# TensorE's job loop entered once with its body skipped, and sixteen turns of the identity at layer 2's begin

## The chip, the cores and the metric

The kernel runs on one core of a Trainium2 chip, as one launch. The metric is the device time of that core in microseconds (us). TensorE, VectorE (DVE), ScalarE (ACT), GpSimd (POOL) and SyncE (SP) each run their own list of instructions and meet at semaphores; TensorE's rows come as PE (matmuls), PEld (weight loads) and a sequencer (rows with q) that waits, branches and loads registers.

## The reference

Three stages, each feeding the next:

```
attention:  q, k of 4 x 12 heads, 448 tokens, 64 wide, RMS-normed; softmax(q k^T / 8) v
            -> x, 1792 tokens x 768
experts:    logits = cos(x, expert_emb) / tau; expert = argmax of 8; gate = its softmax share
            out[mask_e] = gate * (relu(x[mask_e] @ w1[e]) @ w2[e])      # 768 -> 1024 -> 768
layer 2:    (sigmoid(x @ w_gate) * (x @ w_val)) @ w_out                 # 768 -> 1536 -> 768
```

How many tokens an expert gets is known only when attention and routing have run. All is in float32; the kernel makes each product from three products of a high and a low part.

## The kernel before

Each stage is a block: every engine has its own code in it, and all five meet at a barrier between blocks. `attention` (lines 183 to 1040) works through 24 pairs of heads. GpSimd makes its constants (`constants`, line 150) inside this block, one after the other with a wait on each; TensorE there opens with 52 turns of the identity (line 874).

`experts` (line 1198) begins with VectorE's `job_table`, some twenty small instructions that turn the counts per expert into a list of jobs. A job is up to 294 tokens (T) of one expert; there are between 8 and 14 of them, so the loops over jobs have a length that is loaded from the table. Each engine's `jobs` waits for `table_ready` and loads that number. VectorE then clears six PSUM banks (`banks_set`) and waits for `tokens_turned`; TensorE turns the list of tokens (line 1571), VectorE copies it out (line 1476), which releases `tokens_out`, and then scales the gathered rows of the first job (line 1497). TensorE turns these rows into the first job's x (line 1578), ScalarE and VectorE split it into XH and XL, and the first product of line 1539 can start.

TensorE's loop (line 1582) holds the job's code twice: once with 256 columns (TS) for a short job, once with 294 (T) for a long one, 306 matmuls each, one behind the other in its code. `long_job` loads a flag from the table; two branches choose. Behind a short job, the branch of line 1586 skips the whole long body to reach the loop's end.

`layer2` (line 1591) computes gate and value by seven products of half-blocks (Strassen-like), with TensorE's `product` (three products of line 1984 to 1986 for each of three blocks). Its first products wait for BH and BL, the split tokens, that ScalarE and VectorE make block by block; VectorE's adds of line 1793 (`common` and the others) free the four banks `qb`. Before product 5, counted from 0, TensorE waits for the second add.

Of the kernel before, what the change touches and what calls it, by code (L numbers as in the profile page):

```python
# [25 lines left out]
I32 = mybir.dt.int32  # L26
# [15 lines left out]
KD = DM // 128  # L42
T = 294
GATHERS = 3
TS = 256
# [3 lines left out]
LINES = T // GATHERS  # L49
# [4 lines left out]
HALF = SLOTS // 2  # L54
# [89 lines left out]
    return r  # L144


CONSTS = 19


def constants(nc, c, r, pool):  # L150

    done = [0]

    def const(i):
        i.then_inc(r.consts, 1)
        done[0] += 1
        pool.wait_ge(r.consts, done[0])
    exact = dict(allow_small_or_imprecise_dtypes=True)
    J = MAXJOBS
    const(nc.gpsimd.iota(r.rank[:, :, :], [[0, EARLY], [-1, E]], base=E, channel_multiplier=0, **exact))  # L160
    const(nc.gpsimd.iota(r.cap[:, :], [[LINES * CHUNKS, E]], base=0, channel_multiplier=0, **exact))
    const(nc.gpsimd.memset(r.half[:, :], 0.5))
    const(nc.gpsimd.memset(r.ones[:, :], 1.0))
    const(nc.gpsimd.memset(r.tri[:, :], 1.0))
    const(nc.gpsimd.affine_select(out=r.tri[:, :], in_=r.tri[:, :], compare_op=ALU.is_ge, fill=0.0, base=0,
                                  pattern=[[-1, P]], channel_multiplier=1))
    const(nc.gpsimd.memset(c.ones8[:, :], 1.0))
    const(nc.gpsimd.memset(r.mask_e[:, :, :], 1.0))
    const(nc.gpsimd.memset(r.mask_e[:, :, 0], 0.0))
    const(nc.gpsimd.memset(r.mask_l[:, :, :], 1.0))  # L170
    const(nc.gpsimd.memset(r.mask_l[:, :, 0], 0.0))
    const(nc.gpsimd.iota(r.lines[:, :], [[1, ROWS]], base=0, channel_multiplier=0, **exact))
    const(nc.gpsimd.iota(r.slots[:, :], [[1, SLOTS]], base=0, channel_multiplier=0, **exact))
    const(nc.gpsimd.iota(r.token[:, :].rearrange("p (b t) -> p b t", t=NT), [[S, B], [1, NT]], base=0,
                         channel_multiplier=NT, **exact))
    const(nc.gpsimd.iota(c.thr[:, :, :], [[0, E], [T, NT + 3]], base=0, channel_multiplier=0, **exact))
    const(nc.gpsimd.memset(c.thr[:, :, 0], -1.0))
    const(nc.gpsimd.iota(c.jnum[:, :, :], [[1, J + 1], [0, E]], base=0, channel_multiplier=0, **exact))
    const(nc.gpsimd.iota(c.vals[:, 1, :], [[1, E]], base=0, channel_multiplier=0, **exact))
    const(nc.gpsimd.iota(c.vals[:, 3, :], [[CHUNKS, E]], base=0, channel_multiplier=0, **exact))  # L180
    assert done[0] == CONSTS


# [1009 lines left out]
def experts(nc, c, w1, w2, w_l2, w_sums, x_rows, table_of_slots, ids):  # L1193

    R = LINES
    F1, F2 = FE // 128, KD
    J = MAXJOBS
    with ExitStack() as ctx:
        sb, ps, sem = declare(ctx, nc)
        xr, raw1, raw2, W1H, W1L = c.xr, c.raw1, c.raw2, c.W1H, c.W1L  # L1200
# [7 lines left out]
        hb = [ps(f"hb{i}", [128, 512]) for i in range(3)]  # L1208
# [5 lines left out]
        gated_act = sem("gated_act")  # L1214
        gated_dve = sem("gated_dve")
        index_in = sem("index_in")
        dve_table = sem("dve_table")
        table_ready = sem("table_ready")
        tokens_turned = sem("tokens_turned")
        tokens_out = sem("tokens_out")  # L1220
        slots_written = sem("slots_written")
# [20 lines left out]
        def long_job(eng, j):  # L1242
            return eng.value_load(c.table[0:1, bass.ds(j + 2 * (J + 1), 1)], min_val=0, max_val=1)
# [10 lines left out]
        def jobs(eng, wait):  # L1254
            wait(table_ready, 1)
            return eng.value_load(c.table[0:1, 4 * (J + 1):4 * (J + 1) + 1], min_val=E, max_val=J)
# [160 lines left out]
        def _(dve):  # L1417
# [20 lines left out]
            def job_table():  # L1438
# [30 lines left out]
                chain(nc.vector.tensor_scalar(c.tablef[:, 2, :], c.tablef[:, 2, :], float(TS), None, ALU.is_gt))  # L1469
                nc.vector.tensor_copy(c.table[:, :], c.tablef[:, :, :].rearrange("p a j -> p (a j)")).then_inc(table_ready, 1)  # L1470

            job_table()
            for bank in hb + yb:
                nc.vector.memset(bank[:, TS:T], 0.0).then_inc(banks_set, 1)
            dve.wait_ge(tokens_turned, 2)
# [41 lines left out]
        @block.tensor  # L1517
        def _(pe):
            pe.sem_inc(h_done, SPLIT)
            pe.sem_inc(y_done, SPLIT)  # L1520

            def turn(j, kd):
                if kd == 0:
                    pe.wait_ge(gated_act, j + 1)
                    pe.wait_ge(gated_dve, 2 * (j + 1))
                pe.wait_ge(x_lo, KD * j + kd + 1)
                bank = tx[kd % TX]
                for r in range(GATHERS):
                    last = nc.tensor.transpose(bank[:, r * R:(r + 1) * R], xr[0:R, r, kd * 128:(kd + 1) * 128],
                                               c.ident[0:R, 0:R])  # L1530
                last.then_inc(x_turned, 1)

            def product(out, WH, WL, slot, MH, ML, blocks, n, ready=None):

                for k in range(blocks):
                    if ready:
                        ready(k)
                    mh, ml = MH[:, k, 0:n], ML[:, k, 0:n]
                    nc.tensor.matmul(out[:, 0:n], WH[:, slot, k, :], mh, start=(k == 0), stop=False)  # L1539
                    nc.tensor.matmul(out[:, 0:n], WH[:, slot, k, :], ml, start=False, stop=False)  # L1540
                    last = nc.tensor.matmul(out[:, 0:n], WL[:, slot, k, :], mh, start=False, stop=(k == blocks - 1))  # L1541
                return last

            def h(j, f, n):
                pe.wait_ge(h_lo, F1 * j + f + 1)
                pe.wait_ge(w1_lo, 2 * (RAW1 + F1 * j + f + 1))

                ready = (lambda k: pe.wait_ge(x_lo, TX + KD * j + k + 1)) if f == 0 else None
                product(hb[f % HB], W1H, W1L, f % 2, XH, XL, KD, n, ready).then_inc(h_done, 1)

            def y(j, d, n):
                pe.wait_ge(y_hi, F2 * j + d + 1)
                pe.wait_ge(w2_lo, 2 * (RAW2 + F2 * j + d + 1))

                ready = (lambda k: pe.wait_ge(h_lo, HB + F1 * j + k + 1)) if d == 0 else None
                product(yb[d % YB], W2H, W2L, d % 2, HH, HL, F1, n, ready).then_inc(y_done, 1)

            def job(j, n):
                for f in range(F1):
                    h(j, f, n)  # L1560
                for d in range(F2):
                    y(j, d, n)
                    if d == 0:
                        turn(j + 1, 0)
                    if d + 1 < KD:
                        turn(j + 1, d + 1)

            n_jobs = jobs(pe, pe.wait_ge)
            pe.wait_ge(banks_set, HB + YB)
            for part in range(2):  # L1570
                nc.tensor.transpose(hb[2][0:HALF, part * 128:part * 128 + LINES],
                                    c.tokens[0:LINES, part * HALF:(part + 1) * HALF],
                                    c.ident[0:LINES, 0:LINES]).then_inc(tokens_turned, 1)
            pe.wait_ge(tokens_out, 1)
            for a in range(GATHERS):
                pe.wait_ge((gated_dve, gated_act)[a % 2], a // 2 + 1)
                for kd in range(KD):
                    last = nc.tensor.transpose(first_banks[kd][:, a * R:(a + 1) * R], xr[0:R, a, kd * 128:(kd + 1) * 128],
                                               c.ident[0:R, 0:R])
                    if a == GATHERS - 1:  # L1580
                        last.then_inc(x_turned, 1)
            with pe.Fori(0, n_jobs) as j:
                is_long = long_job(pe, j)
                with pe.If(is_long < 1):
                    job(j, TS)
                with pe.If(is_long > 0):
                    job(j, T)


def layer2(nc, c, w_l2, w_sums, ids_dram, out):  # L1590
# [7 lines left out]
    with ExitStack() as ctx:  # L1598
# [361 lines left out]
        def _(pe):  # L1960
# [28 lines left out]
            def rows(chunk, dh, i, part):  # L1989
# [18 lines left out]
                if part:  # L2008
                    mm.then_inc(o_done, 1)

            for chunk in range(6):
                for gi in range(4):
                    for q in range(7):
                        product(chunk, gi, q)
                for dh in range(2):
                    for some in (range(0, OB), range(OB, OB + 1), range(OB + 1, OB + 2), range(OB + 2, TL)):
                        for part in range(2):
                            for i in some:
                                rows(chunk, dh, i, part)
# [6 lines left out]
def build(nc, q, k, v, g_q, g_k, emb, tau, w1, w2, w_gate, w_val, w_out, out):  # L2026
# [4 lines left out]
    with ExitStack() as ctx:  # L2031
# [12 lines left out]
        with ExitStack() as kept:  # L2044
            def far(name, shape, dt=F32):
                return kept.enter_context(nc.sbuf_tensor(name, shape, dt, side="right"))
            c.table = far("table", [1, 5 * (MAXJOBS + 1)], I32)
            c.raw1 = far("raw1", [128, 4, KD, 128])
            c.W1H = far("W1H", [128, 2, KD, 128], F32R)
            c.W1L = far("W1L", [128, 2, KD, 128], F32R)  # L2050
# [70 lines left out]
```

## Time and profile before

| | |
|---|---|
| median of 3 runs | 1154.52 us (1153.01 to 1155.78) |
| the profiled execution's own time | 1155.25 us |
| its span | 1153.8 us |
| TensorE busy in it | 1104.7 us, 96% |
| VectorE, ScalarE, GpSimd busy | 779.7, 597.4, 365.0 us |
| attention ends, first job starts, layer 2's first product | about 330, 343.2, 658.7 us |
| mean granted clock of TensorE | 0.982 |

Times in the rows are counted from the span's start. The 1.45 us between the span and the execution's time lie around the program. The granted clock is 1.00 at 2.4 GHz and 0.50 at 1.2 GHz. A matmul's start is measured and its end modelled, so the rate of starts tells more than the busy time.

### The profile page before, as it was taken

How to read it: one execution, taken by the hardware profiler on the slowest of the kernel's cores; microseconds unless marked ns; L12 is line 12 of the kernel's file. 1: busy time of each engine (PE TensorE's matmuls, PEld its weight loads, DVE VectorE, ACT ScalarE, POOL GpSimd, SP SyncE). 2: the span in 40 equal slices, each digit the busy share in tenths (PEclk: the TensorE clock that was granted, in tenths of full speed). 3: DMA queues.
4: the chain of work that ended last, by engine and by line, in shares of the span. 5: the costliest groups of instructions: out<-in, count | busy, mean ns of one | idle time of the engine just before them, and what ended most of it. 6: DMA issues, size and time to landing. Idle time of an engine off the chain costs nothing. (4 is left out here: it accounts for less than half of the span.)

```text
span 1153.8 us, 21938 instructions
## 1 busy us (share of the span) xinstructions
PE 1104.7 (96%) x7312; PEld 978.3 (85%) x7313; DVE 779.7 (68%) x1416; ACT 597.4 (52%) x1414; POOL 365.0 (32%) x363
## 2 busy tenths in 40 slices
PE   7999999999959899999999899999999999999997
PEld 6566666666649899999999899999999999999997
DVE  5789988788677545565556796475568675574672
ACT  4777777777625555565555663242245343341441
POOL 7798887888421110111011501100003012000002
PEclk9999999999959999999999999999999999999999
DMA  4355565543427667786778433142231334331312
GB/s 124 90 154 146 171 197 142 150 118 104 130 66 200 162 188 180 189 220 170 183 196 218 120 104 102 50 123 76 82 111 56 110 99 150 108 104 48 111 42 96
DMA packets 207779, 149.64 MB, mean 130 GB/s; under 512 B 12446, under 2 KB 203550, under 8 KB 207718
## 3 DMA queue, kind: packets, MB, share of 16 engines
q1 hardware_dynamic: 203910, 133.80, 42.1%
q0 software_dynamic: 3568, 14.82, 4.2%
q8 instruction: 36, 0.59, 0.2%
q10 hardware_dynamic: 240, 0.23, 0.1%
q14 instruction: 25, 0.20, 0.1%
HBM read 128.29 MB, written 20.53 MB: 129 GB/s over the span
## 5 line engine op out<-in xcount | busy, mean ns | idle before, releaser
L1984 PE MATMUL qb<-BH,l_WH 128*128 128x448 f32 x504 | 185.9, 369 | 3.0 <-DVE BL L1854 3.0
L1986 PE MATMUL qb<-BH,l_WL 128*128 128x448 f32 x504 | 185.9, 369 | 0.0
L1985 PE MATMUL qb<-BL,l_WH 128*128 128x448 f32 x504 | 185.9, 369 | 0.0
L1689 ACT ACTIVATE l_WH<-stream 128x384 fp32r<-128x384 f32 x209 | 100.8, 515 | 127.4 <-PE ob L2007 102.4
L1925 POOL TENSOR_TENSOR quads<-quads 128x448 f32<-128x448 f32 x24 | 30.6, 1276 | 381.7 <-DVE quads L1793 381.7
L1793 DVE TENSOR_TENSOR quads<-qb,quads 128x448 f32<-128x448 f32 x168 | 100.1, 619 | 67.6 <-PE qb L1986 67.4
L1789 DVE TENSOR_TENSOR l_WL<-stream,l_WH 128x384 fp32r<-128x384 f32 x209 | 121.3, 599 | 20.4 <-ACT l_WH L1689 20.4
L791 ACT ACTIVATE PR<-sc,negmax 112x448 f32<-112x448 f32 x192 | 121.9, 658 | 0.7 <-DVE negmax L533 0.5
L1539 PE MATMUL hb<-XH,W1H 128*128 128x256 f32 (+1 forms) x384 | 112.7, 294 | 7.4 <-issue 4.0
L1539 PE MATMUL yb<-HH,W2H 128*128 128x256 f32 (+1 forms) x384 | 112.8, 294 | 0.4 <-DVE W2L L1480 0.4
L2005 PE MATMUL ob<-l_WH,GH 128*128 128x384 f32 x336 | 112.5, 335 | 0.4 <-DVE Y L1873 0.4
L533 DVE TENSOR_REDUCE negmax<-sc 112x2 f32<-112x896 f32 x96 | 100.6, 1085 | 17.6 <-PE sc L914 17.0
L2007 PE MATMUL ob<-l_WH,GL 128*128 128x384 f32 x336 | 112.3, 334 | 0.0
L2006 PE MATMUL ob<-l_WL,GH 128*128 128x384 f32 x336 | 112.2, 334 | 0.0
L1541 PE MATMUL hb<-XH,W1L 128*128 128x256 f32 (+1 forms) x384 | 111.7, 291 | 0.0
L1540 PE MATMUL hb<-XL,W1H 128*128 128x256 f32 (+1 forms) x384 | 111.5, 290 | 0.0
L1540 PE MATMUL yb<-HL,W2H 128*128 128x256 f32 (+1 forms) x384 | 109.8, 286 | 0.0
L1541 PE MATMUL yb<-HH,W2L 128*128 128x256 f32 (+1 forms) x384 | 109.7, 286 | 0.0
L1984 PEld LDWEIGHTS qb<-BH,l_WH 128*128 128x128 f32 x504 | 95.1, 189 | 12.3 <-issue 3.2
L1423 DVE TENSOR_TENSOR W1L<-raw,W1H 128x384 fp32r<-128x384 f32 x132 | 67.9, 556 | 51.9 <-ACT W1H L1379 43.7
L1986 PEld LDWEIGHTS qb<-BH,l_WL 128*128 128x128 f32 x504 | 95.0, 189 | 9.4
L1985 PEld LDWEIGHTS qb<-BL,l_WH 128*128 128x128 f32 x504 | 95.0, 189 | 9.1
(251 smaller groups left out, 2536.1 us busy)
## 6 DMA issues: line engine op xcount, KB each, us to landing
raw<-in_moe_w_dram SPq DMA_DIRECT2D x68, 384.0 KB, 5.1
stream<-in_moe_w_dram SPq DMA_DIRECT2D x48, 512.0 KB, 5.1
stream<-w_sums SPq DMA_DIRECT2D x92, 192.0 KB, 2.4
w_sums<-Sb SPq DMA_DIRECT2D x12, 768.0 KB, 6.3
stream<-in_moe_w_out_dram SPq DMA_DIRECT2D x48, 192.0 KB, 2.4
stream<-in_moe_w_val_dram SPq DMA_DIRECT2D x36, 192.0 KB, 3.0
stream<-in_moe_w_gate_dram SPq DMA_DIRECT2D x33, 192.0 KB, 2.6
raw<-in_q_dram SPq DMA_DIRECT2D x24, 224.0 KB, 3.3
```

Source lines behind the costliest of these rows:

```text
L791: nc.scalar.activation(PR[:, h, j, :], sc[j % 2][0:P, h, 0:S], ACT.Exp, bias=negmax[:, s, j, h:h + 1], accum_out=den[:, s, h, j:j + 1]).th ...
L1539: nc.tensor.matmul(out[:, 0:n], WH[:, slot, k, :], mh, start=(k == 0), stop=False)
L1540: nc.tensor.matmul(out[:, 0:n], WH[:, slot, k, :], ml, start=False, stop=False)
L1541: last = nc.tensor.matmul(out[:, 0:n], WL[:, slot, k, :], mh, start=False, stop=(k == blocks - 1))
L1689: nc.scalar.activation(W(c.WH, n), c.stream[:, n % RING, :], ACT.Copy).then_inc(c.w_hi, 1)
L1789: nc.vector.tensor_tensor(W(c.WL, n), c.stream[:, n % RING, :], W(c.WH, n).bitcast(F32), ALU.subtract).then_inc(c.w_lo, 1)
L1984: nc.tensor.matmul(bank, wh, bh, start=(k == 0), stop=False)
L1985: nc.tensor.matmul(bank, wh, bl, start=False, stop=False)
L1986: mm = nc.tensor.matmul(bank, wl, bh, start=False, stop=(k == 2))
L2005: nc.tensor.matmul(bank, GH[:, f, at], W(c.WH, slot), start=(f == 0), stop=False)
L2006: nc.tensor.matmul(bank, GH[:, f, at], W(c.WL, slot), start=False, stop=False)
L2007: mm = nc.tensor.matmul(bank, GL[:, f, at], W(c.WH, slot), start=False, stop=(f == 3))
```

## The change

The constants get one more, `c.passes[0:1, 0:1] = 1`, at the end of GpSimd's list. VectorE raises `passes_known` before the job table, and after it copies the number of jobs into `c.passes[0:1, 1:2]` and raises it again. TensorE's code between the barrier and the loop, and the loop itself, now stand in a loop `go` of two rounds. Each round waits for `passes_known` to reach `go + 1` and loads its number of rounds of the job loop: 1 in the first, the number of jobs in the second. In the first round the turns and the body of the job loop are skipped by branches on `go`. In `layer2`, TensorE begins with sixteen turns of the 128 x 128 identity into bank `ob[0]`, which nothing reads.

```diff
--- before.py
+++ after.py
@@ -144,7 +144,7 @@
     return r
 
 
-CONSTS = 19
+CONSTS = 20
 
 
 def constants(nc, c, r, pool):
@@ -178,6 +178,7 @@
     const(nc.gpsimd.iota(c.jnum[:, :, :], [[1, J + 1], [0, E]], base=0, channel_multiplier=0, **exact))
     const(nc.gpsimd.iota(c.vals[:, 1, :], [[1, E]], base=0, channel_multiplier=0, **exact))
     const(nc.gpsimd.iota(c.vals[:, 3, :], [[CHUNKS, E]], base=0, channel_multiplier=0, **exact))
+    const(nc.gpsimd.memset(c.passes[:, 0:1], 1))
     assert done[0] == CONSTS
 
 
@@ -1216,6 +1217,7 @@
         index_in = sem("index_in")
         dve_table = sem("dve_table")
         table_ready = sem("table_ready")
+        passes_known = sem("passes_known")
         tokens_turned = sem("tokens_turned")
         tokens_out = sem("tokens_out")
         slots_written = sem("slots_written")
@@ -1469,7 +1471,9 @@
                 chain(nc.vector.tensor_scalar(c.tablef[:, 2, :], c.tablef[:, 2, :], float(TS), None, ALU.is_gt))
                 nc.vector.tensor_copy(c.table[:, :], c.tablef[:, :, :].rearrange("p a j -> p (a j)")).then_inc(table_ready, 1)
 
+            dve.sem_inc(passes_known, 1)
             job_table()
+            nc.vector.tensor_copy(c.passes[:, 1:2], c.tablef[:, 4, 0:1]).then_inc(passes_known, 1)
             for bank in hb + yb:
                 nc.vector.memset(bank[:, TS:T], 0.0).then_inc(banks_set, 1)
             dve.wait_ge(tokens_turned, 2)
@@ -1565,26 +1569,31 @@
                     if d + 1 < KD:
                         turn(j + 1, d + 1)
 
-            n_jobs = jobs(pe, pe.wait_ge)
-            pe.wait_ge(banks_set, HB + YB)
-            for part in range(2):
-                nc.tensor.transpose(hb[2][0:HALF, part * 128:part * 128 + LINES],
-                                    c.tokens[0:LINES, part * HALF:(part + 1) * HALF],
-                                    c.ident[0:LINES, 0:LINES]).then_inc(tokens_turned, 1)
-            pe.wait_ge(tokens_out, 1)
-            for a in range(GATHERS):
-                pe.wait_ge((gated_dve, gated_act)[a % 2], a // 2 + 1)
-                for kd in range(KD):
-                    last = nc.tensor.transpose(first_banks[kd][:, a * R:(a + 1) * R], xr[0:R, a, kd * 128:(kd + 1) * 128],
-                                               c.ident[0:R, 0:R])
-                    if a == GATHERS - 1:
-                        last.then_inc(x_turned, 1)
-            with pe.Fori(0, n_jobs) as j:
-                is_long = long_job(pe, j)
-                with pe.If(is_long < 1):
-                    job(j, TS)
-                with pe.If(is_long > 0):
-                    job(j, T)
+            with pe.Fori(0, 2) as go:
+                pe.wait_ge(passes_known, go + 1)
+                n_jobs = pe.value_load(c.passes[0:1, bass.ds(go, 1)], min_val=1, max_val=J)
+                with pe.If(go > 0):
+                    pe.wait_ge(table_ready, 1)
+                    pe.wait_ge(banks_set, HB + YB)
+                    for part in range(2):
+                        nc.tensor.transpose(hb[2][0:HALF, part * 128:part * 128 + LINES],
+                                            c.tokens[0:LINES, part * HALF:(part + 1) * HALF],
+                                            c.ident[0:LINES, 0:LINES]).then_inc(tokens_turned, 1)
+                    pe.wait_ge(tokens_out, 1)
+                    for a in range(GATHERS):
+                        pe.wait_ge((gated_dve, gated_act)[a % 2], a // 2 + 1)
+                        for kd in range(KD):
+                            last = nc.tensor.transpose(first_banks[kd][:, a * R:(a + 1) * R], xr[0:R, a, kd * 128:(kd + 1) * 128],
+                                                       c.ident[0:R, 0:R])
+                            if a == GATHERS - 1:
+                                last.then_inc(x_turned, 1)
+                with pe.Fori(0, n_jobs) as j:
+                    with pe.If(go > 0):
+                        is_long = long_job(pe, j)
+                        with pe.If(is_long < 1):
+                            job(j, TS)
+                        with pe.If(is_long > 0):
+                            job(j, T)
 
 
 def layer2(nc, c, w_l2, w_sums, ids_dram, out):
@@ -2008,6 +2017,8 @@
                 if part:
                     mm.then_inc(o_done, 1)
 
+            for _ in range(16):
+                nc.tensor.transpose(ob[0][:, 0:128], c.ident[:, :], c.ident[:, :])
             for chunk in range(6):
                 for gi in range(4):
                     for q in range(7):
@@ -2045,6 +2056,7 @@
             def far(name, shape, dt=F32):
                 return kept.enter_context(nc.sbuf_tensor(name, shape, dt, side="right"))
             c.table = far("table", [1, 5 * (MAXJOBS + 1)], I32)
+            c.passes = far("passes", [1, 2], I32)
             c.raw1 = far("raw1", [128, 4, KD, 128])
             c.W1H = far("W1H", [128, 2, KD, 128], F32R)
             c.W1L = far("W1L", [128, 2, KD, 128], F32R)
```

TensorE's list between the barrier and the turns of the token list. Before (`table` is the job table, `hb` and `tx` PSUM banks, `xr` the gathered rows):

```order
L190 UNCONDITIONAL_BRANCH
L1517 UNCONDITIONAL_BRANCH
L1256 TENSOR_LOAD table
L1256 ISA x2
L1571 MATMUL hb<-ident,tokens 84x98 x2
L1578 MATMUL tx<-ident,xr 128x98 x2
```

And of the change, at the same place:

```order
L1521 UNCONDITIONAL_BRANCH
L1572 UNCONDITIONAL_BRANCH
L1572 ISA
L1574 ISA
L1574 TENSOR_LOAD passes
L1574 ISA x2
L1575 COMPARE_AND_BRANCH
L1579 MATMUL hb<-ident,tokens 84x98 x2
L1586 MATMUL tx<-ident,xr 128x98 x2
```

The load of the table's entry has become a load of `passes`, with the loop's own steps ahead of it and a branch behind it; the code from L1572 on is passed twice.

TensorE's list at the end of the experts and the begin of layer 2. Before (`qb` are layer 2's banks, `BH` and `BL` the split tokens, `l_WH` the split weights):

```order
L1586 UNCONDITIONAL_BRANCH
L1582 REGISTER_ALU
L1582 COMPARE_AND_BRANCH
L1198 UNCONDITIONAL_BRANCH
L1959 UNCONDITIONAL_BRANCH
L1984 MATMUL qb<-BH,l_WH 128x448
L1985 MATMUL qb<-BL,l_WH 128x448
```

And of the change:

```order
L1595 UNCONDITIONAL_BRANCH
L1590 REGISTER_ALU
L1590 COMPARE_AND_BRANCH
L1572 REGISTER_ALU
L1572 COMPARE_AND_BRANCH
L1199 UNCONDITIONAL_BRANCH
L1968 UNCONDITIONAL_BRANCH
L2021 MATMUL ob<-ident 128x128 x16
L1993 MATMUL qb<-BH,l_WH 128x448
```

The `go` loop's own add and branch stand behind the job loop's, in the part of the code that the branch behind a short job leads to, and the sixteen turns stand ahead of the first product.

## Rows read from the trace of the kernel before

**Rows 1.** The page, section 1: busy time, share of the span, instructions.
```profile
PE 1104.7 (96%) x7312; PEld 978.3 (85%) x7313; DVE 779.7 (68%) x1416; ACT 597.4 (52%) x1414; POOL 365.0 (32%) x363
```

**Rows 2.** Longest waits of TensorE: total us, times, longest.
```profile
PE hb L1571 <- DVE yb L1474: 6.8, 1, 6.8
PE hb L1539 <- issue: 4.0, 1, 4.0
PE hb L1539 <- DVE W1L L1423: 3.1, 4, 1.0
```

**Rows 3.** Line 1586, its sequencer's branch: to 386 us, and after.
```profile
L1586 PEldq COMPARE_BRANCH  x1: 4648/4648/4648, 379.5 to 379.5; - x1
L1586 PEldq COMPARE_BRANCH  x7: 73/212/213, 421.5 to 653.5; - x7
```

**Rows 4.** DMA queue of 16 KB instruction blocks, 378:388 and 390:463: packets, MB, share.
```profile
q8 instruction: 2, 0.03, 1.2%
q8 instruction: 3, 0.05, 0.3%
```

**Rows 5.** Windows of TensorE: us, busy (x matmuls), granted clock, DMA share, GB/s.
```profile
2.00:7.00 5.00, 5.00 (x24) 1.00 0.73 189
7.50:10.00 2.50, 2.50 (x25) 1.00 0.00 0
21.00:24.30 3.30, 3.30 (x19) 0.50 0.52 141
386.20:389.50 3.30, 3.30 (x18) 0.50 0.20 59
390.00:393.30 3.30, 3.30 (x30) 1.00 0.11 32
659.30:662.60 3.30, 3.30 (x11) 0.50 0.54 66
664.00:667.30 3.30, 3.30 (x18) 1.00 0.01 2
```

**Rows 6.** Timeline of TensorE in attention: two waits and what ended them.
```profile
18.64 0.46 PE L914 MATMUL sc<-KH,QH 64*112 64x448 f32 x2 [1.95 <-ACT PR L791]
77.13 0.60 PE L897 MATMUL tqk<-ident,qkn 112*128 112x112 f32 x4 [1.15 <-POOL qkn L305]
```

**Rows 7.** Timeline of GpSimd in its list of constants.
```profile
69.43 0.10 POOL L177 MEMSET thr<- 1x8 f32 x1
69.61 0.30 POOL L178 IOTA jnum<- 1x120 f32 x1
```

**Rows 8.** TensorE's sequencer: last step before the table wait; loop's return, branch on kind.
```profile
L1520 PEldq EVENT_SEMAPHORE  x1: 51/51/51, 331.6 to 331.6; - x1
L1582 PEldq COMPARE_BRANCH  x1: 247/247/247, 384.3 to 384.3; - x1
L1584 PEldq COMPARE_BRANCH  x1: 87/87/87, 385.4 to 385.4; - x1
```

**Rows 9.** Timelines from the job table to the first product, TensorE and VectorE.
```profile
337.15 0.55 PE L1571 MATMUL hb<-ident,tokens 98*84 98x98 f32 x2 [6.77 <-DVE yb L1474]
337.74 0.36 DVE L1476 CAST tokens_T<-hb 84x196 uint32<-84x196 f32 x1 [1.17 <-PE hb L1571]
338.70 0.62 DVE L1497 TENSOR_SCALAR xr<-xr 98x768 f32<-98x768 f32 x1 [0.60 <-issue]
343.20 0.58 PE L1539 MATMUL hb<-XH,W1H 128*128 128x256 f32 x1 [0.19 <-DVE XL L1485]
```

**Rows 10.** Layer 2's begin: barrier; first product; adds of line 1793; first 45 matmuls.
```profile
L1198 PEldq EVENT_SEMAPHORE  x1: 51/51/51, 657.2 to 657.2; - x1
658.71 0.44 PE L1984 MATMUL qb<-BH,l_WH 128*128 128x448 f32 x1 [2.99 <-DVE BL L1854]
L1793 DVE TENSOR_TENSOR quads<-qb,quads x2: 611/613/615, 667.6 to 668.1; 128x448 f32<-128x448 f32 x2
658.70:669.40 10.70, 10.70 (x45) 0.84 0.23 40
```

## The prediction

> **What bounds the kernel now.** I read the page's busy times first: TensorE is busy 1104.7 of 1153.8 us [rows 1], so only what makes it idle, or what makes its matmuls slow, can bring anything. The list of its waits is second, and three of its rows bear on the change: 6.8 us before the turns of the token list, 4.0 us before a product of the experts with "issue" as their cause (no engine is late there), and 3.1 us in four waits for W1L inside jobs [rows 2]. A fourth, 2.99 us at layer 2's first product, stands in the timeline [rows 10]. The rows of line 1586 explain the 4.0: the branch that skips the long body took 4648 ns at 379.5, and 73 to 213 ns in the seven passes after it [rows 3]; job 1 begins right behind the first, and between them the sequencer only closes one round of the loop and opens the next [rows 8]. Within the same ten microseconds the queue of instruction blocks moved two blocks, 0.03 MB [rows 4]. So, as I read it, the first skip leads to code that has not been fetched, and later ones find it there.
>
> Third come the windows at the two levels of the clock. 386.2 to 389.5, right behind the idle 4.04 us, has 18 matmuls at a granted clock of 0.50, which is 1.2 GHz; 390.0 to 393.3 has 30 at 1.00. That is 3.3 x (1 - 18/30) = 1.3 us lost. Behind the 3.0 us of idle before layer 2 it is 11 against 18 matmuls in 3.3 us, again 1.3 us [rows 5].
>
> **The first stall goes.** If round 0 brings the loop's end into TensorE's instruction memory, the branch at the end of job 0 takes about 0.2 us like the seven others, and those are hidden: the sequencer runs ahead of the array, and no wait stands at the other changes of job. 4.0 us go, and with them the 1.3 us at half clock. What is late next is the weight split: four of the short jobs wait for W1L, up to 1.0 us [rows 2], and job 1 was spared because it began late and slow. I give back 0.9. Sum: -4.0 - 1.3 + 0.9 = -4.4.
>
> **Round 0 has a price.** It begins when the table's wait began: the sequencer's last step before it is at 331.6 [rows 8]. From the loop's taken return at 384.3 to the branch on the job's kind at 385.4 it took 1.1 us, of which the return is 0.3 and the loop's head with one table load 0.8 [rows 8]. Round 0 does the same with `passes` (0.8) and, at some 0.1 us each, a first move, a further register step, two moves and 0.3 for a taken branch: 0.15 + 0.1 + 0.1 + 0.8 + 0.3 + 0.2 = 1.65, so the far branch stands at 331.6 + 1.65 = 333.25. It pays the 4.65 us of the first skip [rows 3]: 337.9. Then come two adds and two branches, one of them taken (0.7), the loop's head with the second load (1.0) and the branch and wait before the turns (0.1 to 0.2): 339.7. Before, the turns of the token list began at 337.15 [rows 9]. They are 2.55 us later; I take 2.6.
>
> Nothing hides this. VectorE stands at `tokens_turned` (1.17 us of its idle before 337.74 are TensorE's), and behind it in its own list are the load of the number of jobs, the scaling of the first rows at 338.70, four splits, the second scaling, and then TensorE's turns, ScalarE's XH and the product at 343.20 [rows 9]. All of these follow one another, so 2.6 us at the front are 2.6 at 343.20. The copy into `passes` (0.1 to 0.2 us) and the extra raise of a semaphore on VectorE run in the shade of the fetch; they would cost 0.2 if the fetch were short. SyncE and GpSimd wait for `tokens_out` too, but only to store the list.
>
> From both sides: the table was there one loop's head (0.8) before 337.15, at 336.3, and a fetch that ended by then would cost only some 0.4 us of extra register work; a fetch that has to wait for another block, the one behind the block just entered, costs another 2.3 (half of 4.65) and more, since the gathers of the first rows use the DMA engines at that time. So the price lies between 0.4 and 5, and I take 2.6, the one measured stall.
>
> **The constant.** GpSimd makes its constants back to back: from one memset to the next step it is 69.43 to 69.61, 0.18 us [rows 7]. Its next piece of work ends in the wait of TensorE at 77.13, 1.15 us for `qkn` [rows 6]. One more memset comes through there in full: +0.2.
>
> **Extra branches in the loop.** Each job gets a move and a branch that isn't taken, 0.2 us on the sequencer. It takes the skip of the last job at 653.5 [rows 3], and the array goes on to 658.71 - 2.99 = 655.7 [rows 10]: it is ahead by 2.2. From a skip to the next job's first product it needs 0.2 + 0.1 + 1.1 and three register steps, 1.7. The margin of 0.5 takes the 0.2; at worst it is 0.1 for each of seven changes of job. I take 0.
>
> **Sixteen turns at layer 2's begin.** The barrier opens at 657.2 and the first product waits until 658.71 [rows 10]. At full rate a turn takes 2.5 / 25 = 0.10 to 0.11 us (7.5 to 10.0), at half 0.21 (24 in 5 us) [rows 5]; the sixteen take 1.75 or 3.4 us. At full rate they end at 659.1, 0.4 us past the moment at which the product could start. If the clock stays up, 1.3 us come back: a gain of 0.9. But the sixth product (45 matmuls behind the start, at 669.4) needs the second add of line 1793, done at 668.1 + 0.6 = 668.7 [rows 10], and VectorE works without a pause up to it. So no more than 0.7 arrives. If the clock falls all the same, the turns are lost time: 0.4 us at full rate, up to 3.4 - 1.5 = 1.9 at half. Of idle, 1.6 us are left between 655.7 and 657.3. The nearest rows stand on either side: after 1.95 us of idle before 18.64 the clock was at 0.50 from 21.0 on, after 1.15 us before 77.13 it stayed, which no half clock in the page's slices contradicts [rows 5, 6]. I take 0 between -0.7 and +1.9.
>
> On whether such turns keep the clock at all, the rows speak plainly: from 2.0 to 7.0 TensorE made 24 matmuls, all of them turns of the identity, and 25 from 7.5 to 10.0 [rows 5]; the pace doubled with nothing else running (the clock's column has no record of the first stretch, so its 1.00 there says nothing). The Trainium skill says in "TensorE: Matmul & The Clock Gate", Part 4: PE-mode transpose, that transposes do not count as busy in the same way and do not release the clock. By that page the sixteen turns could only cost; this trace does not agree with it.
>
> **Sum.** -4.4 + 2.6 + 0.2 + 0 = -1.6 us. Against the profiled execution's own 1155.25 us that is 1153.6; its time is 0.7 above the median of 1154.52, so on the scale of the runs I forecast 1152.9.
>
> **Rivals.** A, the round costs nothing that counts: the fetch overlaps the wait for the table, because the memory asks for it sooner than in the one case seen. For it: 4.7 us lie between 331.6 and 336.3. Against: the far branch cannot stand before 333.2. Then -4.4 + 0.4 + 0.2 - 0.5 for the clock kept at layer 2 = -4.3, or 1150.2.
>
> B, the other side: the block is fetched in round 0, but is not there any more at the end of job 0. The place is the branch behind the short body; between round 0 and it, TensorE runs through the whole short body for the first time and brings in its blocks, whereas in the trace of before that body was already there between the first and the second skip. Then the 4.65 us are paid twice and nothing is won: +2.6 + 0.2 = +2.8, or 1157.3; with the turns' cost 1158. It decides from the point at which fewer blocks are held than lie between the loop's head and its end plus those fetched ahead. Against it: the return to the loop's head at 384.3, across both bodies, found its code, and so did all seven later skips, with three blocks fetched between 390 and 463 [rows 3, 4, 8].
>
> The Trainium skill has a rule for it: "Runtime: NRT & Kernel Launch", Instruction fetch mechanics, says that a taken branch whose target isn't in the current window of two pages waits for a fetch. By that rule every job would stall at line 1586, and round 0 could save nothing. The rows with 73 to 213 ns speak against it after the first time.
>
> C, two fetches in a row in round 0: price 5 instead of 2.6, sum +0.8, or 1155.3.
>
> D, the clock falls at layer 2 and the turns run at half rate: -1.6 + 1.5 = -0.1, or 1154.4.
>
> **Chances.** Forecast 0.42 (its own range 1151.6 to 1154.0), A 0.18, B 0.18, C 0.09, D 0.13. The range must leave out no more than 2 in 10: from A's middle, 1149.8, to B's, 1157.3. About 0.2%, 2.3 us, is what a measurement of this kernel can tell from no change. Faster than 1152.2: A, and about four tenths of the forecast's case, 0.36. Slower than 1156.8: most of B and a little of C, 0.18. Between: 0.46.
>
> **What would show it.** In the profile of the changed kernel: two passes of the far branch; the first, at about 333, of 4.6 us, the second, at the end of job 0, of 0.2. The turns of the token list at about 339.7 instead of 337.15, the first product at 345.8. No "issue" wait of 4 us and no half clock behind job 0, but a wait of 0.9 us for W1L in job 1. One q8 block near 335. At layer 2, sixteen turns from 657 less the shift, and matmuls behind them at a granted clock of 1.00 or 0.50, which decides between the forecast and D. A far branch of over 1 us at the end of job 0 makes the forecast wrong and B right; turns of the token list before 338 make it wrong and A right.

## The result: slower by 0.3%, the far skip is paid twice

The changed kernel takes 1157.69 us (median of 7 runs, 1156.11 to 1158.97), the kernel before 1154.52 beside it (7 runs, 1151.59 to 1156.49): a ratio of 1.003, 95% interval 1.0019 to 1.0040, slower by some 3.2 us. I had forecast 1152.9. It is rival B, whose sum was 1157.3. The profiled execution took 1156.96 us, 1155.5 of them the span.

TensorE does the same work in the same time; sixteen turns are added. The page's first section and the waits of TensorE (total us, times, longest), to be held against [rows 1, 2]:

```profile
PE 1104.9 (96%) x7328; PEld 978.6 (85%) x7329; DVE 774.5 (67%) x1417; ACT 598.3 (52%) x1414; POOL 366.5 (32%) x364
```

```profile
PE hb L1579 <- issue: 9.8, 1, 9.8
PE hb L1543 <- issue: 4.6, 1, 4.6
PE ob L2021 <- PEq L1199: 1.6, 1, 1.6
PE qb L1993 <- DVE quads L1802: 0.2, 1, 0.2
```

The wait of 6.8 us for VectorE before the turns of the token list has become 9.8 us with "issue" as its cause, and the 4.0 before job 1 is not gone but 4.6. The sequencer's rows say why. Line 1591 is the condition on the round, line 1595 the skip of the long body (line 1586 before, [rows 3]):

```profile
L1591 PEldq COMPARE_BRANCH  x1: 4867/4867/4867, 336.2 to 336.2; - x1
L1595 PEldq COMPARE_BRANCH  x1: 4891/4891/4891, 384.6 to 384.6; - x1
L1595 PEldq COMPARE_BRANCH  x7: 72/210/215, 427.6 to 655.7; - x7
```

So the branch takes 4867 ns in round 0, near the 4.65 us forecast, and the skip at the end of job 0 takes 4891 ns again. The seven passes after it are short. Two of them are no skips: jobs 2 and 5 are long, so there the branch isn't taken and TensorE runs on into the long body (73 ns at 429.5). Five skips do find their code. The queue of instruction blocks over 335 to 342 us, 362 to 378 (the middle of job 0), 378 to 392 (its end) and 390 to 465 (packets, MB, share; [rows 4] before):

```profile
q8 instruction: 3, 0.05, 3.0%
q8 instruction: 2, 0.03, 1.0%
q8 instruction: 2, 0.03, 0.9%
q8 instruction: 4, 0.07, 0.3%
```

After round 0's three blocks, job 0 brings two more in order while it works, and then its end asks for one again in the midst of the stall; the fourth row counts the one at 391.9 a second time.

The timeline shows both stalls on the array ([rows 9] before):

```profile
342.85 0.52 PE L1579 MATMUL hb<-ident,tokens 98*84 98x98 f32 x2 [9.84 <-issue]
345.13 0.56 PE L1586 MATMUL tx<-ident,xr 98*128 98x98 f32 x2 [1.76 <-DVE xr L1501]
348.94 0.58 PE L1543 MATMUL hb<-XH,W1H 128*128 128x256 f32 x1 [0.25 <-DVE XL L1489]
391.52 0.57 PE L1543 MATMUL hb<-XH,W1H 128*128 128x256 f32 x1 [4.59 <-issue]
```

The barrier ahead of the experts opened at 333.91 (331.28 before), and from there to the first product it is 15.03 us against 11.92: 3.1 later. The rest of what moved shows in the windows ([rows 5, 10]; us, busy, granted clock, DMA share, GB/s) and at layer 2's begin:

```profile
27.80:31.10 3.30, 3.30 (x17) 0.50 0.12 29
393.00:396.30 3.30, 3.30 (x17) 0.50 0.00 0
661.30:671.04 9.74, 9.53 (x48) 1.00 0.18 23
```

```profile
659.61 1.94 PE L2021 MATMUL ob<-ident 128*128 128x128 f32 x16 [1.63 <-PEq L1199]
661.30 0.45 PE L1993 MATMUL qb<-BH,l_WH 128*128 128x448 f32 x1
671.04 0.47 PE L1993 MATMUL qb<-BH,l_WH 128*128 128x448 f32 x1 [0.21 <-DVE quads L1802]
```

Job 1 starts at half clock again (17 matmuls in 3.3 us, as the 18 of before). But the half clock lasts longer: to 396.4, where it had ended 3.4 us after its begin in the kernel before; over 389.7 to 396.3 TensorE starts 22 matmuls at 0.50, against 58 at 1.00 before. In attention there is one more stretch at 0.50, from 27.8, and attention ends 2.6 us later than before. The change isn't needed for that: turns_only below, whose attention is the code of the kernel before, has such a stretch at 28.4. In layer 2 the turns run at full rate (16 in 1.7 us), no stretch at 0.50 follows, the first 45 products take 9.74 us instead of 10.75, and the 46th waits 0.21 us for `quads`.

In this execution the four waits for W1L, 3.1 us before, are absent. So the two spans differ by only 1.7 us: attention +2.6, the start of the experts +3.1, the jobs -3.5 (3.1 of it the waits), layer 2's begin -0.7. The same kernel profiled on another chip has them again:

```profile
PE hb L1543 <- DVE W1L L1425: 2.6, 6, 1.1
```

### The profile page after: what moved, and what is told of

Its sections match the earlier page's. It is cut to its first block and busy times, and to the rows that moved or that the text cites. A ratio compares the mean times of both kernels' runs of the same rounds, so it can differ in the third digit from the quotient of the medians.

```text
span 1155.5 us, 22009 instructions
## 1 busy us (share of the span) xinstructions
PE 1104.9 (96%) x7328; PEld 978.6 (85%) x7329; DVE 774.5 (67%) x1417; ACT 598.3 (52%) x1414; POOL 366.5 (32%) x364
## 5 line engine op out<-in xcount | busy, mean ns | idle before, releaser
L1934 POOL TENSOR_TENSOR quads<-quads 128x448 f32<-128x448 f32 x24 | 30.6, 1277 | 381.2 <-DVE quads L1802 381.2
L1484 DVE TENSOR_TENSOR W2L<-stream,W2H 128x512 fp32r<-128x512 f32 x96 | 68.9, 746 | 47.3 <-ACT W2H L1388 47.3
```

## The experiments

Two explanations of the second stall were in play. **Slot order**: the memory holds blocks in a ring; a block that a jump fetches takes the place behind the last one fetched, and the next blocks that come in order are written over it. **Return**: a block reached by a jump is lost when TensorE goes back to the loop's head, whatever is fetched between. Eleven runs followed, on three chips (after_again and go_again repeat two kernels on another chip); ratios are to the kernel before on the same chip. A third explanation, that the memory is too small for the loop, is met under reversed.

**go_only** and **turns_only**: one half of the change each.

```
go_only:    the changed kernel without
-            for _ in range(16):
-                nc.tensor.transpose(ob[0][:, 0:128], c.ident[:, :], c.ident[:, :])
turns_only: the kernel before, with those two lines
```

> The changed kernel without the sixteen turns at layer 2's begin, so the skipped round alone. If the skipped round costs its 3.1 us at the start and brings nothing back (the branch at the end of job 0 again near 4.9 us, beside one near 4.9 us in round 0), and the turns were worth -0.7 us in the changed kernel, the time is 1157.9 to 1158.8, about 3.9 above the kernel before. Rival: the attention's longer stretch at half clock (2.6 us in the one profiled execution of the changed kernel) is noise and the round costs less: then it is within 1.5 us of the kernel before or at most 2.5 above. The other rival: the turns cost something at layer 2; then this kernel is faster than the changed one, under 1157.

> The kernel before with only the sixteen turns of the identity at layer 2's begin, TensorE's loop as it was. By the two traces the turns keep the granted clock at 1.0 (before: 3.41 us at 0.5 from 659.24), which takes 1.0 us off the first 45 products, and put their own 0.33 us ahead of the first: about -0.7, that is 1153.6 to 1154.1. Rival (my forecast's point estimate): 0.0, the clock's gain is eaten by VectorE's lag at chunk 0. If the turns cost more than they bring: +0.3 to +1.9.

Measured: go_only 1164.07 us, 1.0056 (1.0034 to 1.0078); turns_only 1155.61 us, 0.9989 (0.9970 to 1.0009). The loss comes with the skipped round: both branches stand in go_only's trace, with 5.11 and 5.15 us. The turns' -0.7 lies inside the interval. The round alone looked dearer than the whole change, which the last pair below answers.

**two_landings**: round 0 also loads what lies behind the short body.

```
                 with pe.Fori(0, n_jobs) as j:
                     with pe.If(go > 0):
                         is_long = long_job(pe, j)
                         with pe.If(is_long < 1):
                             job(j, TS)
+                    with pe.If(go > 0):
+                        is_long = long_job(pe, j)
                         with pe.If(is_long > 0):
                             job(j, T)
```

> The changed kernel with the job's two bodies under two conditions of the round instead of one, so that the skipped round lands twice: behind the 256-column body, and then at the loop's end. Slot-order theory (a block fetched by a jump takes the slot behind the last one fetched, and the blocks fetched next in order are written over it): round 0 has now loaded the blocks behind the 256-column body too, so job 0 fetches few or none in order ahead of the end, and the branch at the end of job 0 takes 0.1 to 0.6 us. Return theory (a jumped-to block is dropped when the engine goes back): it takes 4.6 to 4.9 us again. Both expect two branches of 4.6 to 4.9 us in round 0, so the first product 3 to 5 us later than in the changed kernel.

Measured (one run, 1165.41 us). Its sequencer's rows: the first and the second condition on the round (lines 1591, 1595), and the skip of the long body (1597); and the block queue from 336 to 349 us:

```profile
L1591 PEldq COMPARE_BRANCH  x1: 4737/4737/4737, 336.9 to 336.9; - x1
L1595 PEldq COMPARE_BRANCH  x9: 68/68/5129, 341.7 to 664.2; - x9
L1597 PEldq COMPARE_BRANCH  x8: 70/208/222, 391.8 to 665.1; - x8
```

```profile
q8 instruction: 4, 0.07, 2.7%
```

Round 0 stalls twice (4737 ns, and 5129 as the longest of line 1595), and then the skip at the end of job 0, at 391.8, takes 222 ns, the longest of the eight at line 1597. TensorE went back to the loop's head here as well, so the return theory falls; and the code had waited longer than in the changed kernel (49 us from its block at 343.2, against 46 from 338.5), so age isn't the cause either. The queue shows the other side: four blocks in round 0, and none in job 0 (no row for it from 350 to 434 us).

This kernel also pays for its second load of the flag, 0.9 us between its two branches at each job:

```profile
PE hb L1543 <- issue: 5.9, 5, 1.9
```

This and the second stall of round 0 are, roughly, why its time is so long although job 0 ends without a stall.

**reversed**: the long body first, no round ahead.

```
                 is_long = long_job(pe, j)
-                with pe.If(is_long < 1):
-                    job(j, TS)
                 with pe.If(is_long > 0):
                     job(j, T)
+                with pe.If(is_long < 1):
+                    job(j, TS)
```

> The kernel before with the 294-column body first in the loop and the 256-column body second, no round ahead. Job 0 takes the 256-column body. Slot-order theory: the long skip now comes at job 0's head, its block is fetched by the jump (4.6 to 4.9 us there, the first product that much later), the blocks behind it follow in order, and the end of the loop is reached in order: no branch over 1 us at the end of job 0, nor at the head of job 1, where the loop's head is still held. Return theory (a block reached by a jump is lost when the engine goes back to the loop's head): job 1's head skip (if job 1 is of the 256-column kind) takes 4.6 to 4.9 us again.

Measured (one run, 1152.58 us). The skip of the long body at the loop's head, first pass and the others, and the skip of the short body:

```profile
L1584 PEldq COMPARE_BRANCH  x1: 3862/3862/3862, 344.6 to 344.6; - x1
L1584 PEldq COMPARE_BRANCH  x7: 77/208/215, 385.7 to 612.1; - x7
L1586 PEldq COMPARE_BRANCH  x8: 73/76/215, 348.6 to 612.4; - x8
```

One stall, at the head, of 3.86 us where I had expected 4.6 to 4.9, and 215 ns at most afterwards, across seven returns. Its time is like the kernel before's: the stall is moved, not removed. The block queue brings six blocks between 340.7 and 381.2 and then none up to 671, through long and short jobs. So the loop's head and those six are all held at once, and the changed kernel, which had fetched five from its round 0 on when it stalled again, did not run out of room.

**hint_late** and **hint_early**: the kernel before, where one instruction of the short body tells TensorE's sequencer the target of the skip behind it.

```
+                    if mark == ("y", d):        # hint_late: ahead of y 3; hint_early: of h 0
+                        marks[mark] = pe.mark_branch_hint_location()
                     y(j, d, n)
...
-                    job(j, TS)
-                with pe.If(is_long > 0):
+                    job(j, TS, ("y", 3))
+                pe.br_cmp(is_long, 1, on_true="pe_joined", on_false="pe_long",
+                          comp_op="IS_LT").branch_hint(marks["y", 3])
+                with nc.body("pe_long", valid_engines=[pe.engine]):
                     job(j, T)
+                nc.switch_bb("pe_joined")
```

> The kernel before, with the branch behind the 256-column body written out by hand and its target announced to TensorE's sequencer by one prefetch instruction ahead of y block 3 of the 256-column body (about two thirds through job 0's last instruction block boundary). No round ahead of the jobs. If the cost at the end of job 0 is the fetch of the block with the loop's end, and an announced block is fetched beside the work and kept, the branch at the end of job 0 takes 0.1 to 0.6 us in place of 4.65, the stretch at 0.5 behind it goes, and the time falls by 3 to 5 us, to 1149.5 to 1151.5. If the announcement does nothing, or fetches the wrong side, the branch stays at 4.6 to 4.9 and the time within 0.7 us of the kernel before. If the announcement drops the block that comes next in order, a new stall of about 4 us stands inside the body: 1154 to 1159.

> hint_late with the announcement ahead of h block 0 of the 256-column body, before its two block boundaries, instead of ahead of y block 3. Slot-order theory: the announced block is brought in at once and is written over by the blocks that follow in order, as round 0's was in the changed kernel: the branch at the end of job 0 takes 4.6 to 4.9 us. Rival: an announced block is held until its branch: 0.1 to 0.6 us, as in hint_late.

Measured: hint_late 1151.60 us, 0.9942 (0.9921 to 0.9963). Its hint and its skip, and TensorE in the first 3.3 us of job 1:

```profile
L1567 PEldq BRANCH_PREFETCH_HINT  x6: 31/31/55, 374.8 to 642.0; - x6
L1592 PEldq COMPARE_BRANCH  x8: 72/227/385, 383.9 to 651.8; - x8
386.10:389.40 3.30, 3.30 (x29) 1.00 0.58 154
```

The longest skip, job 0's, is 385 ns where it was 4648, no idle time over 0.15 us stands before job 1, and it runs at 1.00 with 29 matmuls where 18 stood in [rows 5]. hint_early (one run, 1148.44 us) gives the same, against what I expected of it (its announcement, its skip, and the block queue from 345 to 386 us):

```profile
L1563 PEldq BRANCH_PREFETCH_HINT  x6: 31/34/55, 345.6 to 611.1; - x6
L1592 PEldq COMPARE_BRANCH  x8: 72/226/385, 382.1 to 647.2; - x8
q8 instruction: 3, 0.05, 0.5%
```

Of its three blocks two come ahead of the skip, at 360.0 and 373.8 (the third follows at 384.2), where the kernel before has two at 357.9 and 371.4 and one more in the stall. So the announced block was not fetched at once, at 345.6, and then written over; it seems to come at 373.8, in the place of the block next in order. hint_late has one of its own at 379.2, 4.4 us behind its announcement and ahead of the skip; this ties the short skip to the announcement, and not to the other way in which the branch is written here. That the block wasn't written over says nothing against slot order, since none in order came behind it before the skip. The block that was left out in hint_early is asked for in the first long job, which fetches four (the first at 421.2) where hint_late's fetches three, and costs a wait there:

```profile
424.48 0.30 PE L1539 MATMUL hb<-XH,W1H 128*128 128x294 f32 x1 [0.47 <-issue]
```

**hint_turn** and **hint_best**: hint_late, and the token list turned ahead of the wait for the job table; hint_best has the sixteen turns as well.

```
+            for part in range(2):
+                nc.tensor.transpose(hb[2]...c.tokens...).then_inc(tokens_turned, 1)
             n_jobs = jobs(pe, pe.wait_ge)
             pe.wait_ge(banks_set, HB + YB)
-            for part in range(2):
-                nc.tensor.transpose(hb[2]...c.tokens...).then_inc(tokens_turned, 1)
...
             job_table()
+            dve.wait_ge(tokens_turned, 2)
+            nc.vector.tensor_copy(tokens_T...).then_inc(tokens_out, 1)
             for bank in hb + yb:
                 nc.vector.memset(bank[:, TS:T], 0.0).then_inc(banks_set, 1)
-            dve.wait_ge(tokens_turned, 2)
-            nc.vector.tensor_copy(tokens_T...).then_inc(tokens_out, 1)
```

> The kernel before with three edits: the branch behind the 256-column body announced ahead of y block 3 (as in hint_late), the token list turned by TensorE ahead of its wait for the job table and copied out by VectorE ahead of its six memsets, and the sixteen turns at layer 2's begin. If all three act: -4.4 to -5.5 (branch and half clock at the end of job 0), -1.0 to -1.3 (VectorE's copy of the tokens starts 1.2 us earlier, and with it the scaling of the first gathered rows and the first product), and -0.7 to -2 (no stretch at 0.5 at layer 2): in all 5.5 to 8 us below the kernel before on the same chip. Rival: the first product waits for gathered rows that land no earlier, so the early turn brings nothing, and the turns nothing: 4 to 5.5 below.

> hint_best without the sixteen turns at layer 2's begin: what stands between this one and hint_best on the same chip is the turns' worth. If they bring the removal of the stretch at 0.5 less VectorE's lag: this one is 0.7 to 2 us slower than hint_best. If they are worth nothing: within 0.5 us of it.

Measured: hint_turn 1146.63 us, 0.9942 (0.9927 to 0.9957); hint_best 1147.10 us, 0.9949 (0.9930 to 0.9968). They are the fastest that ran, and both beat the kernel before; the changed kernel did not run on their chip, but its ratios, 1.003 and 1.0036, lie far off theirs. By their ratios neither beats hint_late. The early turn brings less than its 1.0: in hint_turn's timeline

```profile
649.90:660.60 10.70, 10.70 (x45) 0.84 0.21 35
333.03 0.53 PE L1575 MATMUL hb<-ident,tokens 98*84 98x98 f32 x2 [1.31 <-PEq L190]
339.34 0.56 PE L1584 MATMUL tx<-ident,xr 98*128 98x98 f32 x2 [5.78 <-DVE xr L1497]
341.49 0.59 PE L1584 MATMUL tx<-ident,xr 98*128 98x98 f32 x2 [0.94 <-ACT xr L1402]
343.91 0.58 PE L1539 MATMUL hb<-XH,W1H 128*128 128x256 f32 x1 [0.19 <-DVE XL L1485]
340.50 0.94 ACT L1402 ACTIVATE xr<-xr 98x768 f32<-98x768 f32 x1 [4.80 <-DMA xr<-x_rows,index]
```

the tokens are turned at 333.03, but then the array waits 5.78 us for VectorE's scaled rows and 0.94 for ScalarE's; from the barrier (332.62) to the first product it is 11.3 us instead of 11.9 (11.0 in hint_best). ScalarE itself waits for the gathered rows until 340.50, the last row. I take it that the gathers now set the start; no run moved them. In hint_best the first products of layer 2 run at full clock (9.74 us for 45 in its trace, 10.75 in hint_turn's), and from the end of the last job to the 46th the two traces differ by 0.7, which the medians don't show.

**after_again**, **after_hint**, **go_again**: on one chip, the changed kernel, the same with the hint ahead of y 3, and the same without the turns.

> The changed kernel, unaltered, beside the next two on one chip, as their common measure: about 3 us above the kernel before, as in the first comparison.

> The changed kernel with the branch that skips the 294-column body announced ahead of y block 3 of the 256-column body: round 0 stays and costs what it costs, and the end of job 0 is made what the forecast took it to be, a branch of 0.2 us. If the failed step is the one step that failed, the branch in round 0 stays near 4.9 us, the branch at the end of job 0 takes 0.2 to 0.4 us, the time is 4 to 5.5 us below the changed kernel and 0.5 to 2.5 us below the kernel before (my forecast's sum was -1.6). Rival: round 0 costs more than its 3.1 us (its half clock, later transfers); then it stays within 1 us of the kernel before or above it.

> The changed kernel without the sixteen turns, now on one chip with the changed kernel. On another chip it stood 6.5 us above the kernel before, where the changed kernel had stood 3.5 above on its own; the kernels with and without the turns measured on one chip were equal (1147.10 against 1146.63; and 0.9989 of the kernel before). If the turns are worth nothing: within 0.7 us of the changed kernel. If the stretch at 0.5 at layer 2 that they take away counts: 0.7 to 2 us slower than the changed kernel. If the difference between the chips was real: about 3 us slower.

Measured: after_again 1162.62 us, 1.0036 (1.0020 to 1.0051); after_hint 1157.44 us, 0.9991 (0.9976 to 1.0006); go_again 1164.20 us, 1.0043 (1.0022 to 1.0065). In after_hint round 0's branch and the eight passes of the branch over the long body (six skips) are:

```profile
L1595 PEldq COMPARE_BRANCH  x1: 4867/4867/4867, 337.4 to 337.4; - x1
L1599 PEldq COMPARE_BRANCH  x8: 72/228/373, 386.7 to 655.5; - x8
```

With the failed step repaired and all else as it was, the changed kernel is 5.2 us faster, and 1.3 below the kernel before where my sum had -1.6, though its interval holds no difference too. The changed kernel and go_again overlap: of the larger loss of go_only nothing is left but 1.6 us, within the scatter. go_again also shows that round 0's price follows its branch: 3622 ns this time, and 13.7 us from the barrier (335.42) to the first product, where 4867 ns gave 15.0:

```profile
L1591 PEldq COMPARE_BRANCH  x1: 3622/3622/3622, 337.6 to 337.6; - x1
349.16 0.57 PE L1543 MATMUL hb<-XH,W1H 128*128 128x256 f32 x1 [0.27 <-DVE XL L1489]
```

## Why the prediction was wrong, step by step

- **The first stall goes: -4.4. Wrong, and this is the step that failed:** "if round 0 brings the loop's end into TensorE's instruction memory, the branch at the end of job 0 takes about 0.2 us". Round 0 did bring it in; it was gone when it was wanted, 48 us behind its branch. What displaced it are the blocks that job 0 fetches in order: two_landings, where job 0 fetches none, keeps it; it and reversed exclude the return, and reversed a want of room. The term's size was not the fault: with the branch made short, after_hint is 5.2 us below the changed kernel. hint_late is 0.58% (0.37 to 0.79) below the kernel before, 4.3 to 9.1 us, and by the plain medians 5.2. In the traces jobs 0 and 1 together take 80.5 us before and 75.7 in hint_late, so 4.8 less, near the 4.4. The 0.9 that I gave back to W1L shows as a wait of 1.0 us in job 1 of hint_late and 1.1 of after_hint, and not in hint_early.
- I had read "seven later skips are short" as "a block once fetched stays". They were five skips and two passes into a long body, and of the five only the one at 421.5 [rows 3] came before a long job had brought the loop's end in once more. Before the first skip, moreover, job 0 had already brought the short body in, so between it and 421.5 there was nothing left to fetch in order. The one trace I had held no case of a jump followed by blocks in order, except one that I passed over: the three blocks fetched in the first long job [rows 4], after the end of the loop had been fetched at 381.7. Slot order gives just these three, as blocks behind the long body's start that wrote over the jump's. I had weighed this as rival B at 0.18, and its term that all code was found on the return counted for too much.
- The rule of the Trainium skill that I had set against the forecast ("Runtime: NRT & Kernel Launch", Instruction fetch mechanics: a taken branch outside the current window of two pages waits for a fetch) gives the right sign here and still not the right picture: by it, as I applied it, the five skips from 427.6 on would stall too, and they take 215 ns at most.
- **Round 0's price: +2.6, measured +3.1.** The branch stands at 336.16, 2.25 after the barrier; my sum put it 1.97 behind the barrier (331.28 to 333.25), and its fetch took 4.87 instead of 4.65. No second fetch in a row was waited for (rival C), nor did the wait for the table hide it (rival A).
- **The constant: +0.2.** The memset stands in the list with 0.19 us. Not told apart from noise by any run.
- **Extra branches: 0.** No wait with "issue" stands at the other changes of job: right.
- **The turns: 0 between -0.7 and +1.9.** The traces give -0.7 twice (after; hint_best against hint_turn): the clock stays at 1.00 and `quads` takes its part, as the cap said. In all six traces with the turns no stretch at 0.50 stands at layer 2's begin, but it is absent in two of seven without them too (go_only, hint_early). From the end of the last job to the 46th product it is 13.0 to 13.1 us in the six; of the seven it is 13.1 to 13.2 in those two, 13.7 to 13.9 in three, and 15.0 in hint_late and reversed, where the stretch lasts twice as long. So the turns bring between nothing and 2 us, by what the clock would have done. The medians of three comparisons (-1.2, -1.6 and +0.5 us) don't tell it from nothing.
- **The sum.** Round 0 +3.1, constant +0.2, turns -0.7 to 0, the second stall +0.2 (4.89 against 4.65): +2.8 to +3.5, against 3.2 measured. The longer half clock behind job 0 is not in it. Job 1, from its first product to job 2's, takes 38.5 to 39.4 us in the four profiles in which the skip stalls a second time, and 37.8 and 37.7 in the kernel before and turns_only: 0.7 or more that the prediction had nowhere. Since the waits for W1L and the stretches at 0.50 move by 2 to 3 us from one execution to the next, the fit of this sum is in part luck. So is that of rival B's 1157.3, which has 2.6 for round 0 and nothing for the turns or for job 1. The lower bound of the range, given as A's 1149.8, is 1150.2 by A's own sum; nothing hangs on it.

## What to carry to other kernels

A dry run through a loop loads code, but only code that nothing fetched in order afterwards displaces: count the blocks between where the dry run ends and where the code is wanted, and look for a re-fetch in the trace of before. A far skip that is taken late in a body is better announced in that body: one instruction of 31 to 55 ns took away what a whole extra round could not. And a step that rests on "found once, found always" needs a row in which the same history came before: of the "seven skips" five were skips, and one came before the loop's end was fetched again.

## What the runs showed of the hardware

- A jump to a block that isn't held cost TensorE 3.6 to 5.15 us (fourteen cases in nine traces, twelve of them 4.6 to 5.15). In the queue's records the 16 KB transfer begins 1.1 to 2.7 us behind the branch's start and takes 0.9 to 1.4 us (2.2 in two_landings' second case, with another block under way), and the branch ends 1.4 to 1.6 us behind its landing in all fourteen. The two short ones, go_again's 3.62 and reversed's 3.86, are those whose transfer began early (1.3 and 1.1 us).
- The clock's stretch at 0.50 behind the second stall lasted 6.8 us in after, after_again, go_only and go_again, and 3.4 us behind the only stall of before and turns_only.
- An announcement did its work from either place, some 9 us (hint_late) or 37 us (hint_early) ahead of the branch.
- The memory held seven blocks at once in reversed, and yet lost one after two fetched in order in the changed kernel: room isn't the rule of what goes.
- The slot order is my reading of when blocks are fetched. It fits the counts of all the traces (three blocks again in the first long job wherever a jump ended job 0, four in hint_early, where one had been left out, none in reversed, none in job 0 of two_landings), but the queue does not say which block it moves, so other rules of displacement that spare two_landings stay open.
- The waits for W1L came to anything from 0 to 3.2 us (1.0 in turns_only, 2.6 in after_again, 3.2 in hint_late) in kernels whose jobs are alike: one profile can hide three microseconds of a change in them.
